# Down-sampled attention values: probabilities turned on VectorE, and a TensorE visit of their own in row tiles of 32 keys

## The reference, cut to what matters

```python
q_d = q.reshape(B, H, 144, 4, D).mean(axis=3)      # k_d and v_d likewise
out_d = sm_attn(q_d, k_d, v_d)                     # softmax(q_d k_d^T / 8) v_d, 144 x 144 per head
out_up = np.repeat(out_d, 4, axis=2)
scores = where(|row - column| < 4, q k^T / 8, -1e9)
x = out_up + softmax(scores) v                     # "local" attention
x = ((x @ w1) * (x @ w2) @ w3) @ w_out             # 2304 x 512, inner width 1024
y = maximum(maximum(x @ u1, x @ u2), x @ u3) @ u_out
```

## Time and profile before

| | us |
|---|---|
| median of 3 runs | 676.03 |
| lowest, highest | 675.54, 678.62 |
| the profiled execution | 676.97 |
| its span in the profile | 675.2 |
| TensorE busy in the span | 668.1 |

### The profile page before, as it was taken

How to read it: one execution, slowest core, us unless ns; L and a number is a source line. 1 busy time by engine, 2 the same in 40 slices (tenths; PEclk the granted TensorE clock), 3 DMA queues, 4 the chain that set the end, 5 groups by cost and what they waited for, 6 DMA issues and landing times.

```text
span 675.2 us, 15810 instructions
## 1 busy us (share of the span) xinstructions
PE 668.1 (99%) x6272; PEld 641.4 (95%) x6272; DVE 405.8 (60%) x780; ACT 268.3 (40%) x590; POOL 354.3 (52%) x375
## 2 busy tenths in 40 slices
PE   9999999999999999999999999999999999999998
PEld 8787989999998999999999999999999999999997
DVE  5456665656755653466434574676566766757673
ACT  5474434534444344466445462222431223312230
POOL 5899668866994344454344452133661235803341
PEclk9999999999999999999999999999999999999999
DMA  9885469899857759878999698978399773997632
GB/s 305 263 290 159 146 196 293 242 284 289 233 162 237 237 176 388 287 227 303 314 361 363 244 362 321 414 278 288 118 387 355 230 265 129 347 388 229 244 109 94
DMA packets 93384, 178.14 MB, mean 264 GB/s; under 512 B 8576, under 2 KB 40704, under 8 KB 92544
## 3 DMA queue, kind: packets, MB, share of 16 engines
q1 hardware_dynamic: 93312, 177.15, 77.3%
HBM read 135.69 MB, written 41.42 MB: 262 GB/s over the span
## 4 chain that ended last, share of the span: by engine, by line
PE 98%; DVE 1%; issue 1%; ACT 0%; DVEq 0%
PE psum L979 30%; PE psum L980 29%; PE psum L981 29%; PE psum L1024 3%; PE psum L989 2%; PE psum L1033 2%; PE psum L1012 1%; PE psum L997 1%; PE psum L1109 1%; PE psum L1002 1%; ACT psum L1565 0%; PE psum L1045 0%; DVE gate L1353 0%; PE psum L1048 0%; PE psum L1051 0%
## 5 line engine op out<-in xcount | busy, mean ns | idle before, releaser
L1786 POOL TENSOR_TENSOR second_split<-xy,second_split 128x384 fp32r<-128x384 f32 x99 | 104.1, 1072 | 153.1 <-ACT second_split L1560 153.1
L979 PE MATMUL psum<-second_split,weights_split 128*128 128x384 f32 x402 | 134.6, 335 | 0.0
L980 PE MATMUL psum<-second_split,weights_split 128*128 128x384 f32 x402 | 134.3, 334 | 0.0
L981 PE MATMUL psum<-second_split,weights_split 128*128 128x384 f32 x402 | 134.3, 334 | 0.0
L979 PE MATMUL psum<-weights_split 128*128 128x384 f32 x278 | 93.5, 336 | 0.0
L981 PE MATMUL psum<-weights_split 128*128 128x384 f32 x278 | 92.9, 334 | 0.0
L980 PE MATMUL psum<-weights_split 128*128 128x384 f32 x278 | 92.9, 334 | 0.0
L1786 POOL TENSOR_TENSOR weights_split<-xy,weights_split 128x384 fp32r<-128x384 f32 (+1 forms) x64 | 72.7, 1157 | 17.7 <-ACT weights_split L1560 17.6
L979 PEld LDWEIGHTS psum<-second_split,weights_split 128*128 128x128 f32 x402 | 75.4, 188 | 0.6 <-issue 0.3
L980 PEld LDWEIGHTS psum<-second_split,weights_split 128*128 128x128 f32 x402 | 75.5, 188 | 0.0
L981 PEld LDWEIGHTS psum<-second_split,weights_split 128*128 128x128 f32 x402 | 75.5, 188 | 0.0
(11 more groups left out here) (158 smaller groups left out, 1409.3 us busy)
## 6 DMA issues: line engine op xcount, KB each, us to landing
weights_split<-weights_stream SPq DMA_DIRECT2D x39, 768.0 KB, 5.3
weights_split<-weights_stream SPq DMA_DIRECT2D x54, 512.0 KB, 6.9
weights_split<-gate_weights_stream SPq DMA_DIRECT2D x105, 256.0 KB, 4.8
weights_stream<-attention SPq DMA_DIRECT2D x48, 256.0 KB, 3.9
xy<-wa SPq DMA_DIRECT2D x40, 256.0 KB, 5.5
weights_stream<-attention SPq DMA_DIRECT2D x24, 384.0 KB, 3.8
weights_split<-weights_stream SPq DMA_DIRECT2D x6, 1152.0 KB, 5.1
attention<-v_win SPq DMA_DIRECT2D x16, 384.0 KB, 4.7
```

The lines of the kernel that those rows point to most:

```text
L979: pe.matmul(out, lhs[:, 0], rhs[:, 0], start=first, stop=False, skip_group_check=read_between)
L980: pe.matmul(out, lhs[:, 0], rhs[:, 1], start=False, stop=False, skip_group_check=read_between)
L981: return pe.matmul(out, lhs[:, 1], rhs[:, 0], start=False, stop=last, skip_group_check=read_between)
L1786: return pool.tensor_tensor(out, full, high.bitcast(F32), ALU.subtract)
```

## The change

The down-sampled probabilities stay in PSUM after the division, padded to 5 blocks of 32 keys (three groups of 160 columns). VectorE turns them in 32 x 32 blocks with one instruction of 128 x 480. The query rows are laid out anew (steps of 48 queries, 24 in each block of 32 partitions), so that each block of 32 partitions holds 32 keys of one head and one half of the queries. The visits T are gone. A visit D of 20 matmuls of 72 columns sums the values over the 5 key blocks, in 32 x 64 tiles: two heads times two halves, the halves in banks 6 and 7. It waits for `vd_ready` and the turned probabilities. Its place is piece 11.5, 26.6, 41.5 and 54.5 in units 0 to 3 and 5.5 parts after S later. `copy_up` follows D, and V waits for it. S of unit 1 stands at 19.2, not 17.2. `copy_turned`, the identity matrix and its load go. v comes down in a copy for each half, 128 x 1280 elements and not 80 x 1024, so `v_sum` adds 640 and 320 elements per partition. For units 0 to 3 `load_v4` of the next unit follows S by 8 and not 5.

```diff
-DJ, DROWS, DSTEP, DOWN = 3, 64, 40, 48
+DJ, DAHEAD, DSTEP, DOWN, DROWS = 3, 8, 48, 24, 64
+DB = -(-SD // TW)
+SD_PAD = DB * TW
...
-FIRST_VISITS = {"S": [-0.5, 17.2, 34.5, 47.5], "T": [7.6, 24.2, 40.7, 53.7], "V": [15.2, 31.9, 45.3, 58.3]}
-VISITS = {"S": 0, "T": 5, "V": 7.6}
+FIRST_VISITS = {"S": [-0.5, 19.2, 34.5, 47.5], "D": [11.5, 26.6, 41.5, 54.5], "V": [15.2, 31.9, 45.3, 58.3]}
+VISITS = {"S": 0, "D": 5.5, "V": 7.6}
...
-    "exp_down": ("S", 1), "exp_local": ("S", 2.2), "copy_turned": ("T", 0.1), "copy_up": ("V", 0.9), "v_sum": ("S", 2),
+    "exp_down": ("S", 1), "exp_local": ("S", 2.2), "copy_up": ("D", 0.9), "v_sum": ("S", 2),
...
-        late = {"v_sum": 3.7 if u == 0 else 3.5, "copy_turned": 0.8}.get(name, late)
+        late = {"v_sum": 3.7 if u == 0 else 3.5, "load_v4": 8}.get(name, late)
...
-            def turns(u):
-                pe.wait_ge(down_scaled, u + 1)
...
+            def down_values(u):
+                pe.wait_ge(vd_ready, u + 1)
+                pe.wait_ge(down_turned, u + 1)
+                for b in range(DB):
+                    for h in range(2):
+                        for half in range(2):
+                            first = D * h + TW * half
+                            rows = slice(first, first + min(TW, SD - TW * b))
+                            mm = pe.matmul(pv_down[D * h:D * (h + 1), half, :], vd[rows, b, :], own_rows(rows, b, half),
+                                           start=b == 0, stop=b == DB - 1)
+                mm.then_inc(down_filled, 1)
...
             def values(u):
                 pe.wait_ge(local_turned, u + 1)
+
+                pe.wait_ge(up_ready, u + 1)
                 pe.wait_ge(v_in, 16 * (u + 1))
-                pe.wait_ge(turn_copied, u + 1)
...
-                dve.tensor_tensor(prob_d, score_d, drc.unsqueeze(2).to_broadcast([P, DJ, SD]),
+                dve.tensor_tensor(score_d, score_d, drc.unsqueeze(2).to_broadcast([P, DJ, SD]),
                                   ALU.mult).then_inc(down_scaled, 1)
+                if u == 0:
+                    dve.wait_ge(zeros_made, 4)
+                ge(dve, down_filled, u)
+                dve.wait_ge(down_scaled, u + 1)
+                dve.transpose(prob_d, score_d_all).then_inc(down_turned, 1)
...
+            dve.memset(ahead_of_q, 0.0).then_inc(zeros_made, 1)
             dve.memset(gate[:, 0, 0:P], 0.0).then_inc(zeros_made, 1)
             dve.memset(qk_sb[0:D, 2, :], 0.0).then_inc(zeros_made, 1)
+            dve.memset(score_d_pad, 0.0).then_inc(zeros_made, 1)
...
-            def copy_turned(u):
-                act.wait_ge(down_turned, u + 1)
-                copy(prob_dt, turned_d).then_inc(turn_copied, 1)
```

More of the change, by code:

```diff
@@ L526, in build, with own_rows @@
         v_sb = cut(TG * P).rearrange("p (g c) -> p g c", g=TG)
-        v4_in_sb = cut(2 * FACTOR * P, TD_PAD).rearrange("p (k j c) -> p k j c", k=2, j=FACTOR)
-        v4_sb = v4_in_sb[0:TD]
-        vd = cut(2 * P, TD).rearrange("p (k c) -> p k c", k=2)
+        v4_sb = cut(DB * FACTOR * D).rearrange("p (b j c) -> p b j c", b=DB, j=FACTOR)
+        vd = cut(DB * D).rearrange("p (b c) -> p b c", b=DB)
         prob_t = cut(2 * TG * TW)
[L532 to L537, removed]
+        ahead_of_q = cut(DAHEAD)
+        q_at = used[0]
+        qkd = cut(2 * SD).rearrange("p (a s) -> p a s", a=2)
+        prob_d_at = used[0]
+        prob_d = cut(DJ * SD_PAD)
+        def own_rows(rows, b, half):
+            at = prob_d_at + TW * b + (0 if half else DAHEAD)
+            return att[rows, at:at + DJ * SD_PAD].rearrange("p (j c) -> p j c", j=DJ)[:, :, 0:DOWN]
         up_t = cut(SD)
         mask = cut(TG * TW).rearrange("p (g k) -> p g k", g=TG)
-        ident = cut(P)
         dnb, dsum, drc = (cut(DJ) for _ in range(3))
         lmax, lrc = (cut(2 * TG) for _ in range(2))
-        score_d = bank(6)[:, 0:DJ * SD].rearrange("p (j k) -> p j k", j=DJ)
+        score_d_all = bank(6)[:, 0:DJ * SD_PAD]
+        score_d_pad = score_d_all.rearrange("p (j k) -> p j k", j=DJ)[:, :, SD:SD_PAD]
+        score_d = score_d_all.rearrange("p (j k) -> p j k", j=DJ)[:, :, 0:SD]
         score_by_head = psum[:, 512 * 4:512 * 6].rearrange("p (h c) -> p h c", h=2)[:, :, 0:TG * TW].rearrange(
@@ L571, in prob_of @@
                 "p (h g q) -> p h g q", h=2, g=TG)
[L572 to L576, removed]
+        PV, PV_DOWN = 256, 400
+        pv_down = psum[:, 512 * 6:512 * 8].rearrange("p (n c) -> p n c", n=2)[:, :, PV_DOWN:PV_DOWN + DJ * DOWN]
+        dmax, dsum_eps = (bank(6)[:, DJ * (SD_PAD + i):DJ * (SD_PAD + i + 1)] for i in range(2))
         lsum, lsum_eps = (bank(4)[:, 400 + 2 * TG * i:400 + 2 * TG * (i + 1)] for i in range(2))
@@ L988, in scores @@
                         rows = slice(D * h, D * h + D)
-                        mm = pe.matmul(score_d[rows, j, :], qkd[rows, 0, DSTEP * j:DSTEP * j + DROWS], qkd[rows, 1, :],
+                        at = q_at + DSTEP * j - DAHEAD
+                        mm = pe.matmul(score_d[rows, j, :], att[rows, at:at + DROWS], qkd[rows, 1, :],
                                        start=True, stop=True)
@@ L1027, in values @@
                 mm.then_inc(local_filled, 1)
[L1028 to L1035, removed]
             def first_product(i):
@@ L1712, in gated_y @@
                 copy(y_place(s + 1, j, n), bank(G_BANKS[j])[:, 0:HALF]).then_inc(y_ready, 1)
-            run = {"exp_down": exp_down, "exp_local": exp_local, "copy_turned": copy_turned, "copy_up": copy_up,
+            run = {"exp_down": exp_down, "exp_local": exp_local, "copy_up": copy_up,
                    "SPLIT": split_w, "W3O_OUT": product_high, "SPLIT_X": split_x, "GATE": gate_copy, "H": h_high,
@@ L1717, in _ @@
                    "HIGH_WC": high_wc, "XE": split_xs, "K": keep, "G": gated_high, "GY": gated_y}
-            for step in in_order(unit_jobs(["exp_down", "exp_local", "copy_turned", "copy_up"]), weight_splits(),
+            for step in in_order(unit_jobs(["exp_down", "exp_local", "copy_up"]), weight_splits(),
                                  product_out(), x_splits(), after_parts(["GATE", "H", "Y"]),
```

45 lines of the change are left out of this document (18 added, 27 removed).

## The result

The changed kernel takes 688.03 us (median of 4 runs, 684.64 to 690.85); the kernel before, beside it, 676.81 (675.54 to 678.62). The ratio is 1.0156, 95% interval 1.0128 to 1.0185: 11.2 us slower, where 7.0 were forecast. It lies in the range (674 to 690) and just above the likeliest case's own range (678 to 688). The profiled execution took 689.0 us with a span of 687.2, 12.0 us more than the 677.0 and 675.2 of before.

What follows compares the result with a forecast made beforehand. TensorE, busy 99% of the span, was taken to bound the kernel. Waits at D +11.7, small waits +0.3, later start +0.1 and saving -5.1 gave +7.0 on 676.0: 683.0 us, range 674 to 690.

Steps and rivals of the forecast that it cites:

- the likeliest case's own range: Whole kernel: 678 to 688 us, with D from 0.8 to 1.2 us and waits of 9 to 14 us.
- The wait that D brings: TensorE at D, waiting for GpSimd's longer sums of v, wanted later before: 11.7 us in all.
- the small units: Units other than 0, 2, 3, 5, 7 and 11: waits at D of at most 0.2 us together.
- D's price: Visit D on TensorE: 0.98 us a unit with four tiles together, including 0.20 for leaving.
- two at a time: Rival, D's tiles run in twos: D costs 1.65 us a unit, total 694 us; chance 0.08.
- The saving: TensorE's work: 1.30 us removed and 0.98 added per unit, saving 0.32 a unit, 5.1 us over 16.
- the clock falls in a wait: Rival: TensorE's clock drops to 1.2 GHz at three waits, 4 to 5 us more, 688 us; chance 0.06.
- the clock drops in slices 1 to 4 or 6: Sign that the prediction is wrong: TensorE's granted clock falls in those slices of the changed kernel's profile.
- Turn, sums, copies: VectorE's turn 0.69 us, hidden; GpSimd's sums 1.56 and 0.87 us; V's early copy wait and S's `x_out` wait 0.3.
- The hole of 1.2 us may close or open anywhere: TensorE's one hole before, put down to "issue": it may vanish or appear elsewhere; no term in the sum.
- The sums of v are in time: Rival: GpSimd's sums end within 0.3 us of D's place, leaving only the saving, 671 us; chance 0.13.
- the cover named in the prediction: VectorE's turn is hidden behind the wait for the sums or behind pieces; without that it costs 0.69 us a unit.

Runs made afterwards that it cites:

- the run with the wait alone: The kernel before with one line added, making visit T wait for the sums of v: 695.28 us, ratio 1.0292.
- the run with early sums: The changed kernel with `v_sum` earlier in GpSimd's order and the first unit's D and V later: 680.4 us, ratio 1.0061.
- the waits filled: The changed kernel with matmuls nobody reads put ahead of D's waits in six units: 687.15 us, ratio 1.0179.
- the repairs: Two versions of the changed kernel: D moved right behind V, 680.9 us, and `v_sum` earlier with the first unit's D and V later, 680.4 us.
- another schedule: Early sums with D at 6.5 and the last four units' sums back at S plus 2, 689.29 us; with 160 semaphore instructions added, 684.66 us.
- the kernel before with the shift: The kernel before with 160 semaphore instructions that wait for nothing in TensorE's pieces of w_out @ w3: 681.25 us, ratio 1.0062.
- with D later and 160 instructions: Early sums with D at 6.5, the last four units' sums back at S plus 2, and 160 semaphore instructions added: 684.66 us, ratio 1.0106.
- with 64: Early sums with D at 6.5, the last four units' sums back at S plus 2, and 64 semaphore instructions: 689.37 us, ratio 1.0151.
- the run with the early copy: The kernel with D at 6.5 and 160 semaphore instructions, with `copy_up` at D plus 0.1, not D plus 0.9: 677.68 us, ratio 1.0009.

## Why the prediction was right or wrong

- **The wait that D brings: right, its exact total by luck.** 11.7 us in six waits was forecast, 11.7 in six measured, in the units named. By unit, forecast and measured: 2.2 and 1.69, 1.9 and 1.80, 1.4 and 2.38, 3.1 and 2.92, 1.2 and 1.02, 1.7 and 1.88. Unit 3 is the term that was off, by 1.0: I had set TensorE back by unit 2's wait and let GpSimd stand where it was. Both came later than forecast, TensorE at D by 4.0 us (66.54 against 62.55), the end of the sum by 4.9 (68.86 against 63.95). That the total comes out to 0.1 us is luck, as unit 0 and the small units erred the other way. That the wait by itself makes the kernel slower is shown by the run with the wait alone, and that moving the sums removes it by the run with early sums.
- **D's price: right.** The chain of the changed kernel, unit 4:

```profile
87.67 0.79 PE psum L1017 x40
88.45 0.37 PE psum L981
```

  0.79 and 0.20 of leaving is 0.99 against the 0.98 forecast for four tiles at a time; two at a time would have taken 1.65. By the rule of the Trainium skill (TensorEngine Tiling (Array Packing), Restrictions and Gotchas) on row tiles and banks it would have been these 1.65 us; for outputs on different partitions the measurement decides against it.
- **The saving: a size somewhat off.** By busy time at full clock it is 4.2 us in the changed kernel and 3.9 with early sums, against 5.1. In the run with early sums all 16 visits D take 0.79 us from their first record to the next piece's, so the missing microsecond is not in D; where it is stays open.
- **The clock: the step that failed.** The sum left it out and the rival "the clock falls in a wait" had 0.06, with 4 to 5 us and 688 us. That is what happened: three falls, 5.1 us, and a median of 688.03. By its own sign (the clock drops in slices 1 to 4 or 6) the forecast's mechanism was wrong there: the first fall, 20.0 to 23.4 us, lies in slice 2. The argument was that the trace of before has no idle time over 1.2 us. That made the case untried, and I read it as unlikely. The runs say the falls go with the waits: in the profiled executions the clock is 1.00 with the sums in time, with the waits filled the three places keep it, and with the wait alone on the old kernel it falls three times (a mean of 0.988 to 0.993 in all four executions). It is not all or nothing: two executions with the sums in time have 0.997 and 0.995, and so have some of the kernel before. Which wait draws a fall stays open: 1.69, 2.92 and 1.88 us did and 1.80, 2.38 and 1.02 did not.
- **Turn, sums, copies.** The turn took 683 ns (0.69 forecast), the sums 1558 and 869 (1.56 and 0.87), the wait of S for `x_out` 0.2 (0.3 for both small waits). All right.
- **"The hole of 1.2 us may close or open anywhere": right and too cheap.** In the changed kernel it closed and one of 1.8 opened, so it did not decide the result. In the repairs it decided: 8.2 us and, less V's waits for its copy, 4.7.
- **"The sums of v are in time" would give 671 us: wrong as priced.** With that condition made true the kernel takes 680.4. The price took only the saving and neither new issue waits, nor V's waits for its copy (1.3 us), nor 1.3 us for the turn (the cover named in the prediction gone), nor 1.4 us for the split pushed back.

With the clock put in, the forecast of 683.0 becomes 688; without it the changed kernel would be at 689.0 - 5.1 = 683.9 against a forecast of 684.0 for that execution.

## What to carry to other kernels

When a visit on the engine that sets the time is given an input that was wanted later before, subtract the two times unit by unit: that alone gave the 11.7 us here, while counting instructions gave a gain. New idle time on TensorE should be priced with falls of the clock (three behind six waits of 1.0 to 2.9 us, 1.7 us each here), not left as an unlikely rival because no row shows it. And in a kernel at 98% TensorE, compare schedules only after looking at where the "issue" waits fall: 160 instructions that do nothing made the kernel before 4.3 us slower and another schedule 4.6 us faster by the medians, about 8 at full clock.

## What the runs showed of the hardware that was not expected

- In the schedules without added instructions, TensorE's waits named issue, V's waits for its copy apart, come back at one count modulo 256 of its records (193 or 194), 0.2 to 2.3 us each, 3.6 in the kernel before with the shift; they end 1.2 to 1.6 us after a 16 KB transfer of instructions in nearly all cases. The six of 7.7 us went when only the count was shifted by 160.
- Each fall of the changed kernel's clock lost 1.7 us; twice one lost twice that, with D later and 160 instructions (0.51 and 0.63 in the windows from 164 to 168 and from 168 to 172 us: 1.96 + 1.48 us) and with 64 (0.62 and 0.53 from 120 to 124 and from 124 to 128 us). The length of the wait does not decide alone: one of 2.38 us ahead of 68.92 had no fall behind it, one of 1.23 us ahead of 100.68, in the run with the early copy, had.
- A wait for a copy from another engine can be named issue, and one at a count of 195 modulo 256 can be named after GpSimd. What told them apart was to shift the count, after which the first kind stayed with its visit and the second with its count, and the last transfer of q8: 1.46 us ahead of the restart at record 707, 5.8 to 9.0 us ahead of V's three starts with 160 instructions.
